# A delta-rule attention feeding two feed-forward layers: how the first two chunks' triangular inverses are computed, and where the later stages sit in the units

## The reference

```python
def _attn_ref(q, k, v, beta):                       # B=4, H=8, S=768, D=48
    k_n = k / (np.linalg.norm(k, axis=-1, keepdims=True) + 1e-06)
    for t in range(S):
        y[:, :, t] = np.einsum('bhd,bhde->bhe', q[:, :, t], state)
        v_old = np.einsum('bhde,bhd->bhe', state, kt)
        state = state + bt[:, :, :, None] * np.einsum('bhd,bhe->bhde', kt, vt - v_old)
...
h = np.maximum(x @ w_in, 0.0);  x = h * h @ w_out             # 3072 x 384, d_ff 2048
...
out = silu(x @ w_gate) * (x @ w_val) @ w_out2                 # d_ff 1536
```

## Time and profile before

| | |
|---|---|
| profiled execution, its own time | 1036.29 us |
| its span | 1034.5 us |
| TensorE busy | 972.1 us (94%) |
| VectorE, ScalarE, GpSimd busy | 415.5, 306.7, 216.3 us |
| first matmul of the first unit | 67.46 us after the start |
| mean granted TensorE clock | 0.997 |

### The profile page before, as it was taken

How to read it: one execution, slowest core, us unless ns; L and a number is a source line. 1 busy time by engine, 2 the same in 40 slices (tenths; PEclk the granted TensorE clock), 3 DMA queues, 4 the chain that set the end, 5 groups by cost and what they waited for, 6 DMA issues and landing times.

```text
span 1034.5 us, 24141 instructions
## 1 busy us (share of the span) xinstructions
PE 972.1 (94%) x10692; PEld 807.2 (78%) x10692; DVE 415.5 (40%) x693; ACT 306.7 (30%) x599; POOL 216.3 (21%) x342
## 2 busy tenths in 40 slices
PE   2179899999999999999999999999999999999998
PEld 2168789778777877877888888888888888888887
DVE  3976644634643554453266422321321312312222
ACT  2225333332433332332255421211211211212211
POOL 1188283482284087000000000000000000000000
PEclk9999899999999999999999999999999999999999
DMA  6656657456344523612153100100100100100000
GB/s 217 196 158 179 170 149 182 111 129 162 98 118 121 148 72 99 139 68 54 32 204 132 50 12 1 61 1 1 62 1 1 61 1 1 62 1 1 31 1 30
DMA packets 115544, 85.67 MB, mean 83 GB/s; under 512 B 89776, under 2 KB 94512, under 8 KB 115440
## 3 DMA queue, kind: packets, MB, share of 16 engines
q1 hardware_dynamic: 109776, 76.79, 26.3%
q10 hardware_dynamic: 5664, 7.34, 2.3%
HBM read 63.14 MB, written 20.97 MB: 81 GB/s over the span
## 4 chain that ended last, share of the span: by engine, by line
PE 91%; DVE 4%; DMA 2%; issue 1%; ACT 1%; ACTq 0%; SPq 0%; DVEq 0%
PE bank L1059 91%; DVE first_tinv L463 1%; DVE first_prod L460 1%; DVE h_lo L1018 1%; DMA tri_scratch<-gram 0%; DMA first_tri<-tri_scratch 0%; DMA k_dim<-in_kt 0%; ACT h_hi L782 0%; DVE w_lo L997 0%; DMA inv_scratch<-first_tinv 0%; DMA inv<-inv_scratch 0%; ACT gram L804 0%; DVE norm L924 0%; ACT k_sq L815 0%; PE bank L1233 0%
## 5 line engine op out<-in xcount | busy, mean ns | idle before, releaser
L1059 PE MATMUL bank<-x_hi,w_hi 128*128 128x512 f32 (+1 forms) x768 | 293.2, 382 | 1.2 <-DVE x_lo L993 1.2
L1059 PE MATMUL bank<-x_lo,w_hi 128*128 128x512 f32 (+1 forms) x768 | 289.2, 377 | 0.0
L1059 PE MATMUL bank<-x_hi,w_lo 128*128 128x512 f32 (+1 forms) x768 | 289.1, 376 | 0.0
L1059 PE MATMUL bank<-h_hi,w_hi 128*128 128x512 f32 (+1 forms) x552 | 211.4, 383 | 4.1 <-DVE h_lo L1018 3.1
L1059 PE MATMUL bank<-h_hi,w_lo 128*128 128x512 f32 (+1 forms) x552 | 205.1, 372 | 4.2 <-issue 4.2
L1059 PE MATMUL bank<-h_lo,w_hi 128*128 128x512 f32 (+1 forms) x552 | 205.0, 371 | 0.0
L1038 DVE TENSOR_TENSOR stage<-bank,stage 128x512 f32<-128x512 f32 x72 | 49.8, 692 | 318.5 <-ACT stage L889 318.5
L1059 PEld LDWEIGHTS bank<-x_hi,w_hi 128*128 128x128 f32 x768 | 144.9, 189 | 28.9 <-DVE x_lo L993 1.5
L1059 PEld LDWEIGHTS bank<-x_hi,w_lo 128*128 128x128 f32 x768 | 144.9, 189 | 26.4
L1059 PEld LDWEIGHTS bank<-x_lo,w_hi 128*128 128x128 f32 x768 | 145.0, 189 | 25.4
L1012 DVE TENSOR_TENSOR stage<-stage,bank 128x512 f32<-128x512 f32 (+1 forms) x112 | 68.5, 612 | 195.2 <-ACT stage L861 194.9
(11 more groups left out here) (98 smaller groups left out, 559.3 us busy)
## 6 DMA issues: line engine op xcount, KB each, us to landing
w_raw<-in_w SPq DMA_DIRECT2D x12, 576.0 KB, 3.7
k_dim<-in_kt SPq DMA_DIRECT2D x12, 512.0 KB, 4.6
q_dim<-in_qt SPq DMA_DIRECT2D x12, 512.0 KB, 4.0
k_prep<-in_kt SPq DMA_DIRECT2D x10, 512.0 KB, 4.3
x1s<-in_w ACTq DMA_DIRECT2D x12, 384.0 KB, 5.1
k_sq<-in_ky SPq DMA_DIRECT2D x12, 384.0 KB, 3.6
v_tok<-in_vy SPq DMA_DIRECT2D x12, 384.0 KB, 3.1
x_in<-x_scratch SPq DMA_DIRECT2D x6, 768.0 KB, 5.0
```

The source lines that it names most:

```text
L1059: return pe.matmul(dst, lhsT, rhs, start=start, stop=stop, **kw)
```

## The change

It does the following.

- **Chunk 0** (prologue): no triangles, no trip through DRAM. GpSimd makes masks (`pairs`) for blocks of 1, 2, 4, 8 and 16. VectorE weights the masked Gram matrix (stages sums, weights, S), TensorE adds it to a unit matrix (I, B), and four levels double the block: T (eight 128x128 transposes), E (unit matrix plus the cut-out part times the inverse so far), L (product); a last T follows. Every I, T, E and L takes two PSUM banks; T, E, L are copied out half by ScalarE, half by VectorE. GpSimd's `cut` makes the cut-out part for each level. Key weights come from squares of k_tok on ScalarE.
- **Chunk 1**: four 16x16 blocks (`store_small`, eight transfers), 15 columns on VectorE laid between the levels of chunk 0 (`cols`); `second_blocks` takes them through DRAM (one store, eight loads), and in unit 0 V, I, E, L, T (slots 1, 3, 3, 5, 7) join them.
- **Weights** 0 to 6: the low part and the scaling of v of chunk 0 move from VectorE to GpSimd, ahead of the solve of pair 1, which begins after the lane stage of pair 1, now in slot 0 of unit 0 (before: in the prologue).
- **Unit 0**: the square is on ScalarE.
- **Transfers** of q, k, prepared k are two of 48 partitions each, without the zeros.
- **Plan**: N1, N2 and U of pair 1 go from unit 0 (slots 26, 28, 32) to unit 1 (10, 12, 14); chunks 2 and 3 follow there (Y 3 in slot 26, was 12; DS 3 in 28, was 15). Pair 2's N1 is in slot 13 of unit 2 (was 1), Y 5 in 27 (was 21). Pair 3's N1 is in slot 3 of unit 3 (was 32 of unit 2). From unit 4 on the plan is as before.
- **SyncE's queue** is reordered with it. `store_inverses(1)` stands behind `store_x1(0)`, and `store_inverses(3)` behind `store_x1(2)`.

```diff
+        PE_FIRST = [("G", 0), ("G", 1), ("I", 0), ("B", 0), ("I", 1), ("T", 1), ("E", 1), ("L", 1), ("I", 2), ("T", 2),
+                    ("E", 2), ("L", 2), ("I", 3), ("G", 2), ("T", 3), ("E", 3), ("L", 3), ("I", 4), ("G", 3), ("T", 4),
+                    ("E", 4), ("L", 4), ("T", 5), ("QK", 0), ("U", 0), ("Z", 0), ("DZ", 0), ("Y", 0), ("DS", 0),
+                    ("X", 0, 0), ("X", 0, 1)]
...
+        DVE_FIRST = [("sums", 0), ("sums", 1), ("weights", 0), ("S", 0), ("B", 0), ("T", 1), ("E", 1),
+                     ("L", 1), ("T", 2), ("E", 2), ("root", 0), ("L", 2), ("lane", 0), ("T", 3), ("solve", 0), ("E", 3),
+                     ("cols", 0, 2), ("L", 3), ("cols", 2, 3), ("T", 4), ("E", 4), ("cols", 3, 5), ("L", 4),
+                     ("cols", 5, 6), ("T", 5), ("cols", 6, 9), ("QK", 0), ("U", 0), ("cols", 9, 12), ("Z", 0),
+                     ("cols", 12, 15), ("DZ", 0), ("Y", 0), ("DS", 0), ("X", 0, 0), ("X", 0, 1)]
...
             elif u == 1:
+                put(10, "N1", 1)
+                put(12, "N2", 1)
+                put(14, "U", 2)
...
+                put(23, "U", 3)
+                put(24, "G", 7)
+                put(26, "Y", 3)
+                put(28, "DS", 3)
...
+            elif u == 2:
...
+                put(27, "Y", 5)
+                put(29, "DS", 5)
...
+                    if t == 3:
+                        put(3, "N1", t)
...
             store_x1(0)
+            store_inverses(1)
+            load_inverses(1)
+            load_triangles(2)
             load_q(3)
+            store_y(2)
             load_ktok(3)
-            store_y(2)
+            load_ky(5)
+            load_x(2)
             load_v(4)
             load_k(4)
-            load_ky(5)
-            load_x(2)
             load_prep(7)
-            store_both(6)
             load_q(4)
             store_y(3)
             load_ktok(4)
+            store_both(6)
             load_prep(8)
+            load_x(3)
             store_both(7)
...
+            load_x(4)
+            load_q(6)
+            store_both(9)
+            load_prep(10)
+            store_y(5)
+            load_ktok(6)
+            load_x(5)
...
+            for u in range(3, NIT):
...
                 store_x1(u - 1)
+                if t == 3:
+                    store_inverses(t)
+                    load_inverses(t)
+                    load_triangles(p)
...
+            cut(1)
+            pool.memset(small_inv[:, :, :], 0.0).then_inc(small_zeroed, 1)
+            cut(2)
             pool.memset(inv[:, 16:32, :], 0.0).then_inc(inv_zeroed, 1)
             pool.memset(tinv[:, :, :], 0.0).then_inc(tinv_zeroed, 1)
-            pool.wait_ge(dve_sub_step, SUB)
+            cut(3)
+            low(pool, 0)
+            cut(4)
+            scale(pool, 0)
+            low(pool, 1)
+            cut(5)
+            for f in range(2, RING + SPARE):
+                low(pool, f)
...
+                elif name == "E":
+
+                    pe.wait_ge(unit_filled, n + 1)
+                    pe.wait_ge(level_cut, n)
+                    for ready in level_ready:
+                        pe.wait_ge(ready, n + n // (LEVELS + 1))
+                    for r in range(2):
+                        for a in range(4):
+                            for bp in range(2):
+                                for ab in range(2):
+                                    at = (4 * r + a) * C
+                                    done = mm(pair[bp][toks(ab), at:at + C], cut_out(n)[toks(bp), r, 2 * a + ab, :],
+                                              level_x[toks(bp), 4 * r + a, ab, :], start=False, stop=True,
+                                              skip_group_check=True)
+                    done.then_inc(rest_filled, 1)
```

More of the change, by code:

```diff
@@ L11, in program @@
     AX = mybir.AxisListType
[L15 removed]
+    NCH, P = kt.shape[0], 128
     C, HALF, D = 64, 32, 48
@@ L235, in plan @@
             if u == 0:
[L236 to L261, removed]
-            elif u == 1:
[L263 to L267, removed]
+                for f in range(RING + SPARE, NF1):
+                    put(2 * f - 6, "w1", f)
+                    put(2 * f - 5, "low", f)
@@ new lines, in plan @@
+                put(0, "lane", 1)
+                put(1, "V", 0)
+                put(2, "sq", 1)
+                put(3, "I", 5)
+                put(3, "E", 5)
+                put(4, "root", 1)
+                put(5, "L", 5)
+                put(6, "scale", 1)
+                put(7, "T", 6)
+                put(8, "KS", 1)
+                put(9, "QK", 1)
+                put(10, "sq", 2)
+                put(11, "U", 1)
+                put(13, "Z", 1)
+                put(14, "G", 4)
+                put(14, "root", 2)
@@ new lines, in columns @@
+        def columns(eng, a, x, products, size, steps, at, first, last):
+            for j in range(first, last):
+                block = [P, j + 1, size - 1 - j]
+                share = products[:, 0:block[1] * block[2]].rearrange("p (c i) -> p c i", i=block[2])
+                eng.tensor_tensor(share, a[:, j:j + 1, j + 1:size].to_broadcast(block),
+                                  x[:, 0:j + 1, j:j + 1].to_broadcast(block), ALU.mult).then_inc(steps, 1)
+                eng.wait_ge(steps, at + 2 * j + 3)
+                below = x[:, 0:j + 1, j + 1:size]
+                eng.tensor_tensor(below, below, share, ALU.add).then_inc(steps, 1)
+                eng.wait_ge(steps, at + 2 * j + 4)
@@ L677, in _ @@
             load_ktok(4)
+            store_both(6)
             load_prep(8)
+            load_x(3)
             store_both(7)
-            load_x(3)
+            store_x1(1)
+            load_v(5)
+            load_ky(6)
+            load_k(5)
             store_inverses(2)
@@ L683, in _ @@
             load_triangles(3)
-            for u in range(2, NIT):
+            load_q(5)
+            load_ktok(5)
+            store_y(4)
+            load_ky(7)
+            load_prep(9)
+            store_both(8)
+            load_v(6)
+            load_k(6)
+            load_x(4)
[6 more added lines that the diff above has]
+            for u in range(3, NIT):
                 t, p, g = u, u + 1, u + 2
@@ L1336, in by_dim @@
     def by_dim(x):
-        out = np.zeros((n, 2, 64, 2, 4, 2, t), x.dtype)
-        out[:, :, :d] = parts(x).transpose(4, 3, 6, 0, 2, 1, 5)
-        return out.reshape(n, 128, 16 * t)
+        return parts(x).transpose(4, 3, 6, 0, 2, 1, 5).reshape(n, 2, d, 16 * t)
     def columns(w):
```

487 lines of the change are left out of this document (356 added, 131 removed), and 5 rows, old and new, of the table ACT_FIRST.

## The result

The changed kernel takes 1076.03 us (median of 4 runs, 1070.87 to 1077.15) against 1036.45 us on the same chip: ratio 1.0372, 95% interval 1.0336 to 1.0409. It is slower by 3.7%. The forecast was 1049 us with a range of 1025 to 1062: the direction holds, the size does not, and the time lies outside the range. The profiled execution spans 1075.4 us against 1034.5, so 40.9 us are to be found. TensorE is still 94% busy: that share says nothing of the loss, since the span grew with it.

A forecast was written before the change was run, and what follows sets the result against it. TensorE, 94% busy, was taken as the bound, through the first unit's start and waits behind it. 1036.3 - 12.5 (prologue) + 4.6 (stages) + 19.8 (waits) + 4.2 (clock) - 3.2 (gap) gave 1049 us, range 1025 to 1062.

The forecast's parts named there:

- The prologue: Stretch ahead of the first unit: U at 40.6 and the first unit at 55.0, 12.5 us earlier.
- one slow level: Prologue levels: one at the slow TensorE rate (7.3 us) and three at the fast rate (5.0 us each).
- 1.8 for such meetings: Prologue: 1.8 us added for VectorE instructions slowed beside GpSimd products, from w_lo at 1.49 each instead of 0.97.
- A first unit beyond 60: Sign that would show the forecast wrong: the first unit starting later than 60 us instead of near 55.
- The stages: Unit 0: added V, E, L, I and T cost TensorE 4.6 us.
- The four waits: TensorE waits at N1 of pairs 1 and 3 and y of chunks 3 and 5, set by SyncE's order: 19.8 us.
- The wait of 3.4: Unit 1: N1 of pair 1 waits 3.4 us for its blocks, 5.6 us taken from inverse store to `load_cross`.
- +4.2 forecast for two places: Slow clock behind the waits of 5.4 (y of chunk 3) and 8.0 (N1 of pair 3): 4.2 us.
- the gap of 4.23: Wait without a releaser inside a unit of the earlier trace; may return or fall inside a transfer wait: -3.2 us taken.
- Transfers sooner: Faster rival: transfers land sooner in SyncE's chain, waits 8.3 us or wholly covered, total 1035.6 or 1025; chance 0.25.
- The clock stays low in the levels: Rival: all prologue levels run at the slow rate, adding 9 to 12 us, total 1060; chance 0.11.
- GpSimd is the bound: Prologue rival: VectorE holds GpSimd up, so X waits for the low parts; 3 to 5 us, total 1053; chance 0.09.

The follow-up runs named there:

- e4_lows_dve: Changed kernel with low parts 0 to 6 and the scaling of v back on VectorE, column steps 7 to 14 behind the first X, chunk 1's stages later: 1070.77 us.
- e8_no_five: Changed kernel without the five stages V, I 5, E 5, L 5 and T 6 that join chunk 1's blocks: 1067.46 us.
- e2_nocols: Changed kernel without 30 of VectorE's column steps of chunk 1 in the prologue: 1067.57 us (one execution).
- e3_earlier_y: Changed kernel with stages of chunks 3 and 5 one to three slots earlier and their y ahead of the triangles in SyncE's queue: 1069.13 us.
- e1_queue3: Changed kernel with pair 3's inverse stores and loads ahead of unit 2's x in SyncE's queue: 1071.95 us.
- e10_fill_n1: Changed kernel with 30 filler matmuls of 128x512 ahead of N1 of pair 3, where TensorE waited: 1071.84 us.
- e11_fill_two: e10_fill_n1 with 26 more filler matmuls ahead of the last down group of unit 1: 1068.66 us.
- e5: e4_lows_dve's prologue with G 5 behind Z of chunk 1, and from the end of unit 0 the order of the kernel before the change: 1059.03 us.
- e9: e5 without the five stages that join chunk 1's blocks: 1055.18 us.
- e6: Changed kernel with the edits of e1_queue3, e3_earlier_y and e4_lows_dve together, G 5 behind Z of chunk 1: 1065.32 us.

## Why the prediction was wrong

The error is 28.0 us in the profiles (+12.9 forecast, +40.9 measured in the span), 27 in the medians. It has two places.

**The prologue, 18.1 of it: -12.5 forecast, +5.6 measured.** This is the step that failed. By milestones:
- Up to T 1, 3.5: forecast 14.4, measured 17.92. G 0 starts 0.8 later. I, which I had taken at 0.45, takes 2.08 slow and 1.13 fast. B takes 3.68 where I had the 1.99 of any 64-matmul stage. In the twelve profiles with the change it takes 2.34 to 3.68, and the trace's record of the granted clock, at 1.00, begins while it runs where it is short and at its end where it takes 3.68 (16.41 in the changed kernel). Why even then it is slower than the 1.99 of other stages was not tried by itself; it writes the same half of the partitions that it reads, while E and L write both halves.
- T 1 to U, 12.9: forecast 26.2, measured 39.05. I had one slow level and "1.8 for such meetings" of VectorE and GpSimd. The rate was better than forecast at first, the meetings far worse. I had scaled's w_lo, 1.49 instead of 0.97, and missed that a short step loses just as many microseconds as a long one: four steps that take 0.2 each elsewhere took 6.6 us. e4_lows_dve, with the same levels, needs 29.1 from T 1 (16.70) to U (45.82), 9.9 less. Of these 7.0 fall behind the start of E 3 and are the meetings and the slow clock behind them. Another 2.8 are the slow stretch behind the gap of 2.57, which has nothing to do with VectorE: from the gap's end to E 3 the changed kernel takes 6.2, e4_lows_dve 3.4, and e8_no_five, with the changed kernel's prologue and a gap of 1.49, 3.4 as well. e2_nocols shows that without the column steps the first unit starts 6.2 to 9.2 us earlier.
- U to the first unit, 1.7: forecast 14.4, measured 16.1.
"A first unit beyond 60" was what I had said would show it wrong. The kernel of e4 reached 60.0, so 55.0 would have been too low by 5 even with the meetings gone. Over the seven profiles with this prologue the start moved by +2.7 to +5.6, none of them near -12.5. One reading under it was only half right as well: the six transposes of X take 1.31 together, which is the slow rate, and only the last of them ran at the fast one.

**Units 0 to 4, 9.9 of it: +25.4 forecast, +35.3 measured.** The stages: 4.6 forecast, 5.7 measured; right, and e8 bears it out (6.8 with their waits). The four waits: 3.4, 5.4, 3.0 and 8.0 forecast; 1.07, 5.90, 3.42 (1.17 + 2.25) and 6.65 measured, 17.0 for 19.8. The mechanism and three of four sizes were right, and e3_earlier_y and e1_queue3 take three of them away by order of the queue and the slots, though a gap came up in the place of each of the two longer ones. The wait of 3.4 (its own bounds are 2.9 to 4.2, with 3.55 in the middle) came out as 1.07 since from the inverse store to `load_cross` 4.0 us passed (142.50 to 146.49) and not the 5.6 of the trace before. What was too small is the clock: +4.2 forecast for two places, while the busy time that is not stages grew by 8.6; e10_fill_n1 and e11_fill_two give 3.0 for each of these two, and a third place was not forecast, behind a gap of 2.55 without a releaser at 110.48:

```profile
110.50:118.00 7.50, 7.50 (x169) 6.88 (x172) 1.55 (x2) 3.92 (x10) 6.64 (x12) 0.60 0.39 109
```

At 0.60 over 7.5 us, 3.0 are lost there too. The wait of 2.02 at 126.98 left the clock at 1.00. And the gap of 4.23, for which I had taken off 3.2 as likely to be gone, was replaced by others of the same kind: 7.5 us in units 0 to 4 against 6.8 before. So the 9.9 are made up of: stages +1.1, the four waits -2.8, slow clock +4.4, the gaps +3.9 (the 3.2 taken off and 0.7 more), and +3.3 of other waits that were not forecast, among them 2.00 for k_prep and 2.02 for h_lo.

**The rivals.** "Transfers sooner" did not come: 17.0 of waits, not 8.3. "The clock stays low in the levels" was wrong as written, the first levels were fast in this trace (T 1.07, E 1.16, L 1.16, one after another), and later ones were slow behind a stop only (T 3 1.97, L 4 1.99, T 5 1.94). So the sentence of the Trainium skill on transposes (TensorE: Matmul & The Clock Gate, "Part 4: PE-mode transpose") is not borne out as a reason for slow levels here, since a T stood in each; the small matmuls around it may be what kept the clock up. "GpSimd is the bound" named the right pair of engines and the wrong victim: it was VectorE's steps that stood still, and TensorE's copies behind them.

**What stays open.** Why units 0 and 1 cost 24 us more in e5 and 20 us more in e9 than before is shown only as a sum of waits under 4 us and slow clock; no one cause was isolated. A single profile is a weak witness there: unit 0 of e4 and of e6 differ by the slot of G 5 alone and take 73.1 us at a clock of 0.95 and 79.4 at 0.85. None of the versions beats the kernel before.

## What to carry to other kernels

Before giving GpSimd two-operand work "because it is idle", look at what VectorE does meanwhile: here a chain of short steps on VectorE paid the whole length of a GpSimd instruction at each step. Price a wait of TensorE with the slow stretch behind it, here 3 us for a wait of 6, and expect a start that is won early to be asked back by the queues unless their order moves with it. An average rate from a long instruction is no price for a short one.

## What the runs showed of the hardware

- TensorE stands still when its instructions come late. Twenty gaps of over 2 us without a releaser stand in the thirteen traces (2.08 to 4.92 us). Each of them ends 1.24 to 1.75 us behind the end of a transfer of 16384 bytes of the queue q8, which itself takes 0.9 to 1.5 us, so a gap is long where the transfer began late. The number of these transfers goes with TensorE's matmul and weight-load records: 84 for 21384 before, 91 for 23064 after, 89 for 22656 without the five stages, one for some 254. That is why such gaps stand at fixed places of the program: in L of level 2 always behind the 59th of 64 matmuls, in all twelve profiles with the change, with lengths of 1.28 to 3.12 us. Most of these transfers cause no gap. Why some begin late no run shows, and the shorter gap ahead of Y of chunk 0 (1.93 at 67.37, 1.18 before the change) does not fit them.
- Matmuls that compute nothing, put into 6 us of idle time, saved 3.0 us of slow clock at each of two places.
